# An attention and feed-forward kernel: row-sum reciprocals widened by VectorE into a buffer and turned by four whole transposes

## The chip, the cores and the metric

The kernel runs on one core of one Trainium2 chip. The metric is the device time of one execution in microseconds. Three runs of the kernel before gave 667.19, 667.30 and 667.51 us, median 667.3 us.

## The reference, cut to what matters

```python
q_rot, k_rot = rotate(q), rotate(k)            # (4, 8, 576, 64) float32
scores = scale * q_rot @ k_rot.T               # per batch and head: 576 x 576
attn = exp(scores - max(scores))
attn = attn / (sum(attn) + 1e-9)               # one row sum for each query
x = (attn @ v) -> (2304, 512)                  # heads side by side
h = x @ w_in                                   # (2304, 2048)
g = max(h, 0) + alpha * min(h, 0)
out = g @ w_out                                # (2304, 512)
```

## The kernel before, in words

There are two stages: attention up to about 260 us of the profile, and then the feed-forward products, chunk by chunk. The change is in attention alone.

**Pairs and periods.** Two heads are worked on together; 4 batches of 4 such pairs give 16 pairs. The code counts periods, `p` = 0 to 16. In period p the scores of pair p are computed, the probabilities of pair p are begun to be turned, and the rest of pair p-1 (its turned probabilities, its product with the values, its division by the row sums) is finished. Period 0 has no earlier pair, period 16 no pair of its own. Batches 1 and 2 (periods 4 to 11) run in a loop on all engines but TensorE.

**Tiles.** A pair has 9 score tiles of 128 rows by 576 keys: tile 0 holds the 64 last queries of both heads (`REM_TILE`), tiles 1 to 4 (`A_TILES`) the others of the first head, 5 to 8 (`B_TILES`) those of the second. TensorE computes a tile (`score`, L598) into one of two pairs of PSUM banks. VectorE copies it to SBUF and takes the row minimum of the negated scores (`maxima`, L996). ScalarE takes the exponential and the row sum into a column of `rsum` (`exps`, L828). A tile's banks are free again once its `maxima` is done.

**Units in four banks.** Everything that TensorE turns goes through four PSUM banks in a fixed order of 15 units in each period (`UNITS`, `BANK_OF`). `fill` waits until the unit that was in the bank before has been taken out (the semaphore `evac` of that bank), TensorE fills it, and ScalarE or VectorE takes it out: `flat` (L871 on ScalarE, L1046 on VectorE), `hi` (L847, ScalarE), `lo` (L1021 and L1026, VectorE). `U_MIXED` and `U_INV` follow one another in bank 2, so `U_INV` can't begin before `lo(p, U_MIXED, t)` is done.

**The row sums.** At the start of period p VectorE adds 1e-9 to the nine row sums of pair p-1 (`reciprocals` step 0, L1056) and takes the reciprocal (step 1, L1060) into `inv`, [128 queries, parity, 9 tiles]. To divide, the reciprocals are needed along the free dimension, the same in each of the 64 rows of a head. In `spread`, unit `U_INV`, TensorE gets this with 8 products: the stationary operand is one column of `inv` read 64 times (a step of zero), the moving operand is the 128x128 identity, and the output is one head's half of the bank (L647). The two halves `HEADS` are the two column groups of the array. ScalarE copies the bank to `inv_sb`, and `normalise` (L1071, VectorE) multiplies the product with the values (`pv`, L696 and L700) by it. Tile 0's reciprocals go through `U_MIXED` (L655) and L1026.

**Order.** Each engine runs its own list in order; nothing is reordered between engines but by semaphores. TensorE's period is: KQREM, score 0, QREM, KREM, PB0-1, scores 1 and 2, PB2-3, Q, K, scores 3 and 4, MIXED, `pv` half 0, scores 5 and 6, INV, PA0-1, scores 7 and 8, PA2-3, `pv` half 1. `pv` half 1 reuses the bank of half 0 and waits until `normalise` of half 0 is done.

**GpSimd** rotates the queries and keys of later pairs (`rope`: L453 twice, L458, L462, all with SBUF operands), and in periods 4 to 11 splits `w_in` beside it (L468, L475). L458 on the queries waits until TensorE has done `U_MIXED` (L655).

Of the kernel before, what the change touches and what calls it, by code (L numbers as in the profile page):

```python
# [8 lines left out]
ALU = mybir.AluOpType  # L9
# [3 lines left out]
P = 128  # L13
# [20 lines left out]
def build(nc, q, k, v, w_in, w_out, alpha, cos, sin, eye, out):  # L34
# [27 lines left out]
    def has_prev(p):  # L62
        return not (isinstance(p, int) and p <= 0)
# [34 lines left out]
    def unit_count(p, u):  # L98
        return tally(p, u, range(UNITS))
# [43 lines left out]
    with ExitStack() as ctx:  # L143
        used = [0]

        def sb(stack, name, shape, dt=F32):
            used[0] += -(-4 * int(np.prod(shape[1:])) // 32) * 32
            return stack.enter_context(nc.sbuf_tensor(name, shape, dt))

        def sem(name):  # L150
            return ctx.enter_context(nc.semaphore(name))
# [17 lines left out]
        with ExitStack() as att:  # L169
            rot_q = sb(att, "rot_q", [P, ST, P])  # L170
            rot_k = sb(att, "rot_k", [P, ST, P])
            cos_sb = sb(att, "cos_sb", [P, ST, D])
            sin_sb = sb(att, "sin_sb", [P, ST, D])
            q_nat, q_swap, k_nat, k_swap = [], [], [], []
            for i in range(2):
                q_nat.append(sb(att, f"q_nat{i}", [P, 2, QT * P + P], F32R))
                if i == 0:
                    early = used[0]
            for i in range(2):
                q_swap.append(sb(att, f"q_swap{i}", [P, 2, QT * P], F32R))  # L180
                k_nat.append(sb(att, f"k_nat{i}", [P, 2, REM + S], F32R))
                k_swap.append(sb(att, f"k_swap{i}", [P, 2, HALF], F32R))
            under_w_out = 4 * (2 * CT * CHUNK + FT * DM + 2 * CHUNK)
            sb(att, "behind_scores", [P, (under_w_out - used[0]) // 4])
            of_scores = used[0]
            raw_v = [sb(att, f"raw_v{i}", [P, ST, P]) for i in range(2)]
            sb(att, "behind_values", [P, CT * CHUNK - 2 * ST * P])


            until_prob = used[0]  # L190
            prob = sb(att, "prob", [P, QT, 2 * S])
            prob_rem = sb(att, "prob_rem", [P, S])

            pt = sb(att, "pt", [P, 3 * QT + 1, S])
            inv_sb = sb(att, "inv_sb", [P, S])
            nmax = sb(att, "nmax", [P, 2, TILES])
            rsum = sb(att, "rsum", [P, 2, TILES])
            inv = sb(att, "inv", [P, 2, TILES])
            ident = sb(att, "ident", [P, P])
            zero = sb(att, "zero", [P, 1])  # L200
            tiny = sb(att, "tiny", [P, 1])
            blank = sb(att, "blank", [P, P])
# [67 lines left out]
        evac = [sem(f"evac{i}") for i in range(T_BANKS)]  # L270
        sum_done = sem("sum_done")
        inv_done = sem("inv_done")
        pv_done = sem("pv_done")
        x_done = sem("x_done")
        w_in_high = sem("w_in_high")
# [33 lines left out]
        def is_opening(p):  # L309
            return isinstance(p, int) and p == 0  # L310
# [224 lines left out]
        def _(pe):  # L535
# [92 lines left out]
            def spread(p, t, u):  # L628

                if not exists_now(p, u):  # L630
                    return
                bank = fill(p, u)
                if u == U_KQREM:
                    pe.wait_ge(exp_done, (p - 1) * TILES + 1)
                elif u != U_INV and has_next(p):
                    turned_in(p, 1)
                if u != U_KQREM and has_prev(p):
                    pe.wait_ge(inv_done, p)
                pe.sem_inc(pair_filled, 1)
                par = (t - 1) % 2  # L640
                if u == U_KQREM:
                    for r in HEADS:
                        mm = nc.tensor.matmul(bank[r, 0:REM], prob_rem[:, QT * P:S], ident[:, r], start=True, stop=True)  # L643
                elif u == U_INV:
                    for i in range(QT):
                        for r, n in zip(HEADS, (A_TILES[i], B_TILES[i])):
                            mm = nc.tensor.matmul(bank[r, i * P:(i + 1) * P], inv[:, par, n:n + 1].to_broadcast([P, D]),  # L647
                                                  ident[:, :], start=True, stop=True)
                else:
                    if has_next(p):  # L650
                        for r in HEADS:
                            mm = nc.tensor.matmul(bank[r, 0:P], rot_q[:, QT, r], ident[:, :], start=True, stop=True)  # L652
                    if has_prev(p):
                        for r in HEADS:
                            mm = nc.tensor.matmul(bank[r, P:P + REM], inv[:, par, 0:1].to_broadcast([P, D]),  # L655
                                                  ident[:, r], start=True, stop=True)
                mm.then_inc(turned, 1)
# [324 lines left out]
        def _(dve):  # L982

            def maxima(p, t, n):

                if not has_now(p):
                    return
                dve.wait_ge(scored, p * TILES + (n + 1))
                if has_prev(p):
                    if n == REM_TILE:  # L990
                        dve.wait_ge(turned, unit_count(p, U_QREM))
                    elif n == A_TILES[0]:
                        dve.wait_ge(turned, unit_count(p, U_KREM))
                    elif n == B_TILES[0]:
                        dve.wait_ge(turned, unit_count(p, U_PB[-1]))
                nc.vector.tensor_scalar(row_of(n), s_ps[(t * TILES + n) % 2], -SCALE, None, ALU.mult, ALU.min,  # L996
                                        accum_out=nmax[:, t % 2, n:n + 1]).then_inc(max_done, 1)
# [48 lines left out]
                    ins = nc.vector.tensor_copy(dst, src)  # L1046
                ins.then_inc(evac[BANK_OF[u]], 1)

            def reciprocals(p, t, step):

                if not has_prev(p):
                    return
                par = (t - 1) % 2
                if step == 0:
                    dve.wait_ge(exp_done, p * TILES)
                    nc.vector.tensor_tensor(rsum[:, par, :], rsum[:, par, :], tiny[:, :].to_broadcast([P, TILES]),  # L1056
                                            ALU.add).then_inc(sum_done, 1)
                else:
                    dve.wait_ge(sum_done, p)
                    nc.vector.reciprocal(inv[:, par, :], rsum[:, par, :]).then_inc(inv_done, 1)  # L1060

            def normalise(p, b, t, h):

                if not has_prev(p):
                    return
                n = (p - 1) * 2 + h
                dve.wait_ge(pv_done, n + 1)
                if h == 0:
                    dve.wait_ge(evac[BANK_OF[U_INV]], evac_count(p, U_INV))
                half = slice(h * HALF, (h + 1) * HALF)  # L1070
                nc.vector.tensor_tensor(x[:, t, bass.ds(b * S + h * HALF, HALF)], value_bank(p, h), inv_sb[:, half],  # L1071
                                        ALU.mult).then_inc(x_done, 1)
# [38 lines left out]
            def period(b, t):  # L1111

                p = b * PAIRS + t
                before = (b if t else b - 1, (t - 1) % PAIRS)
                reciprocals(p, t, 0)
                flat(p, U_KQREM, t)
                maxima(p, t, REM_TILE)
                reciprocals(p, t, 1)
                flat(p, U_PB[1], t)
                maxima(p, t, A_TILES[0])  # L1120
                maxima(p, t, A_TILES[1])
                flat(p, U_PB[3], t)
                if not has_now(p):
                    dve.wait_ge(alpha_in, 16)
                    gate(0, 0, 0)
                    low_w_out(0)
                maxima(p, t, A_TILES[2])
                if not is_opening(p):
                    lo(p, U_Q, t)
                if is_closing(p):  # L1130
                    for j in range(CT):
                        split_x(0, 0, j)
                if not is_opening(p):
                    lo(p, U_K, t)
                maxima(p, t, A_TILES[3])
                if not is_opening(p):
                    lo(p, U_MIXED, t)
                maxima(p, t, B_TILES[0])
                maxima(p, t, B_TILES[1])
                if is_opening(p):  # L1140
                    for u in OF_NEW:
                        lo(p, u, t)
                normalise(p, *before, 0)
                maxima(p, t, B_TILES[2])
                maxima(p, t, B_TILES[3])
                flat(p, U_PA[2], t)
                normalise(p, *before, 1)

            nc.vector.memset(blank[:, :], 0.0).then_inc(blank_done, 1)
# [71 lines left out]
```

## Time and profile before

| | |
|---|---|
| median of the three runs | 667.3 us |
| the profiled execution | 667.3 us, its span 665.5 us |
| TensorE (PE) | 654.6 us busy, 98% |
| VectorE (DVE) | 338.2 us busy, 51% |
| ScalarE (ACT) | 320.3 us busy, 48% |
| GpSimd (POOL) | 266.8 us busy, 40% |
| granted TensorE clock, mean | 0.995 |

Between the first and last recorded instruction lie 665.5 us; 1.8 us of the execution lie around it. PE is TensorE's products and transposes, PEld its loading of the stationary operand, which overlaps. An fp32 product leaves two records of its matmul, a transpose or an fp32r product one. Ends of matmuls are modelled, so on PE the distance from start to start is read and not the duration.

### The profile page before, as it was taken

How to read it: one execution, taken by the hardware profiler on the slowest of the kernel's cores; microseconds unless marked ns; L12 is line 12 of the kernel's file. 1: busy time of each engine (PE TensorE's matmuls, PEld its weight loads, DVE VectorE, ACT ScalarE, POOL GpSimd, SP SyncE). 2: the span in 40 equal slices, each digit the busy share in tenths (PEclk: the TensorE clock that was granted, in tenths of full speed). 3: DMA queues.
4: the chain of work that ended last, by engine and by line, in shares of the span. 5: the costliest groups of instructions: out<-in, count | busy, mean ns of one | idle time of the engine just before them, and what ended most of it. 6: DMA issues, size and time to landing. Idle time of an engine off the chain costs nothing.

```text
span 665.5 us, 14995 instructions
## 1 busy us (share of the span) xinstructions
PE 654.6 (98%) x5570; PEld 561.9 (84%) x5570; DVE 338.2 (51%) x779; ACT 320.3 (48%) x730; POOL 266.8 (40%) x254
## 2 busy tenths in 40 slices
PE   7899999999999999999999999999999999999998
PEld 6787778778877777988899999999999999999996
DVE  4577887778887773456423332333233323332222
ACT  2688888888888884333332223222322232223223
POOL 3756788888776214222222222222222222222222
PEclk9799999999999999999999999999999999999999
DMA  6596455445545426000010001000100010001001
GB/s 150 147 230 175 112 127 134 116 105 121 119 107 118 97 91 253 1 0 1 1 49 0 1 0 48 1 1 0 47 0 0 0 47 0 0 0 48 1 0 48
DMA packets 73309, 41.58 MB, mean 62 GB/s; under 512 B 59812, under 2 KB 64292, under 8 KB 72740
## 3 DMA queue, kind: packets, MB, share of 16 engines
q1 hardware_dynamic: 72978, 40.62, 23.3%
q8 instruction: 40, 0.66, 0.4%
q10 hardware_dynamic: 274, 0.16, 0.1%
q14 instruction: 17, 0.14, 0.1%
HBM read 22.95 MB, written 4.72 MB: 42 GB/s over the span
## 4 chain that ended last, share of the span: by engine, by line
PE 96%; DVE 1%; ACT 1%; DMA 0%; SPq 0%; issue 0%; POOL 0%; DVEq 0%
PE banks L756 30%; PE banks L785 30%; PE banks L700 9%; PE banks L598 9%; PE banks L674 5%; PE banks L625 3%; PE banks L696 3%; PE banks L572 2%; PE banks L647 2%; PE banks L652 1%; PE banks L553 1%; DMA cos_sb<-in_cos 0%; PE banks L580 0%; PE banks L655 0%; PE banks L643 0%
## 5 line engine op out<-in xcount | busy, mean ns | idle before, releaser
L520 POOL TENSOR_TENSOR g_lo<-g,g_hi 128x384 fp32r<-128x384 f32 (+1 forms) x98 | 99.7, 1017 | 304.8 <-ACT g_hi L941 301.5
L1105 DVE TENSOR_SCALAR g<-banks,alpha_sb 128x384 f32<-128x384 f32 (+1 forms) x98 | 59.7, 609 | 249.2 <-ACT pos L932 249.2
L756 PE MATMUL banks<-x_hi,w_in_lo 128*128 128x384 f32 x384 | 129.3, 337 | 0.0
L756 PE MATMUL banks<-x_hi,w_in_hi 128*128 128x384 f32 x384 | 129.3, 337 | 0.0
L756 PE MATMUL banks<-x_lo,w_in_hi 128*128 128x384 f32 x384 | 129.0, 336 | 0.0
L932 ACT ACTIVATE pos<-banks 128x384 f32<-128x384 f32 x96 | 47.2, 491 | 169.2 <-PE banks L756 169.2
L785 PE MATMUL banks<-w_out_hi,g_hi 128*128 128x512 f32 x288 | 114.9, 399 | 0.3
L785 PE MATMUL banks<-w_out_hi,g_lo 128*128 128x512 f32 x288 | 112.9, 392 | 0.0
L785 PE MATMUL banks<-w_out_lo,g_hi 128*128 128x512 f32 x288 | 111.9, 389 | 0.0
L941 ACT ACTIVATE g_hi<-g 128x384 fp32r<-128x384 f32 (+1 forms) x98 | 50.9, 519 | 116.5 <-DVE g L1108 116.5
L828 ACT ACTIVATE prob<-prob,nmax 128x576 f32<-128x576 f32 x128 | 98.3, 773 | 1.3 <-DVE prob L996 1.1
L996 DVE TENSOR_SCALAR_CACHE_REDUCE prob<-banks 128x576 f32<-128x576 f32 x128 | 92.8, 751 | 9.6 <-PE banks L598 8.1
L756 PEld LDWEIGHTS banks<-x_hi,w_in_hi 128*128 128x128 f32 x384 | 72.2, 188 | 3.8
L756 PEld LDWEIGHTS banks<-x_lo,w_in_hi 128*128 128x128 f32 x384 | 72.2, 188 | 3.5
L871 ACT ACTIVATE pt<-banks 128x512 f32<-128x512 f32 x112 | 61.6, 595 | 25.0 <-PE banks L625 19.9
L756 PEld LDWEIGHTS banks<-x_hi,w_in_lo 128*128 128x128 f32 x384 | 72.2, 188 | 0.0
L598 PE MATMUL banks<-k_nat,q_nat 64*128 64x288 f32 x375 | 68.4, 314 | 0.1
L598 PE MATMUL banks<-k_swap,q_swap 64*128 64x288 f32 x375 | 67.7, 312 | 0.0
L700 PE MATMUL banks<-pt,raw_v 128*64 128x288 f32 x512 | 67.6, 406 | 0.0
L785 PEld LDWEIGHTS banks<-w_out_hi,g_lo 128*128 128x128 f32 x288 | 54.0, 187 | 13.8
L785 PEld LDWEIGHTS banks<-w_out_hi,g_hi 128*128 128x128 f32 x288 | 54.0, 188 | 10.0 <-issue 1.8
L785 PEld LDWEIGHTS banks<-w_out_lo,g_hi 128*128 128x128 f32 x288 | 54.1, 188 | 8.4
(80 smaller groups left out, 918.2 us busy)
## 6 DMA issues: line engine op xcount, KB each, us to landing
q_swap<-q_nat SPq DMA_DIRECT2D x32, 256.0 KB, 3.8
k_swap<-k_nat SPq DMA_DIRECT2D x32, 144.0 KB, 3.2
out<-stage SPq DMA_DIRECT2D x18, 256.0 KB, 2.0
raw_q<-in_q SPq DMA_DIRECT2D x32, 128.0 KB, 2.9
raw_k<-in_k SPq DMA_DIRECT2D x32, 128.0 KB, 2.6
raw_v<-in_v SPq DMA_DIRECT2D x32, 128.0 KB, 2.3
w_in_raw<-in_moe_w_in SPq DMA_DIRECT2D x4, 1024.0 KB, 6.9
w_out_raw<-in_moe_w_out SPq DMA_DIRECT2D x8, 512.0 KB, 6.9
```

Source lines behind the costliest of these rows:

```text
L520: nc.gpsimd.tensor_tensor(g_lo[f % 2][:, part], g[f % 2][:, part], g_hi[f % 2][:, part].bitcast(F32), ALU.subtract).then_inc(g_lo_done, 1)
L598: mm = nc.tensor.matmul(tile[:, h, :], q_of[rows, qx, of_q], k_of[rows, kx, keys], start=(j == 0), stop=(j == len(SPLIT) - 1))
L674: mm = nc.tensor.transpose(bank[:, to:to + D], prob[r, i, first + w * P:first + (w + 1) * P], ident[r, r])
L700: mm = nc.tensor.matmul(o[own, :], raw_v[par][:, j, own], pt[:, pt_slot(par, head, j), cols], start=False, stop=(j == QT - 1))
L756: mm = nc.tensor.matmul(h_ps[f % 2], w[:, j, cols], xx[:, j, :], start=(step == 0), stop=(step == 3 * CT - 1))
L785: mm = nc.tensor.matmul(y_ps[c % 2][m], lhs[j][f % 2][:, m * P:(m + 1) * P], rhs[j][:, f, :], start=(f == 0 and j == 0), stop=(f == FT - 1 ...
L828: nc.scalar.activation(row_of(n), row_of(n), ACT.Exp, scale=-1.0, bias=nmax[:, t % 2, n:n + 1], accum_out=rsum[:, t % 2, n:n + 1]).then_in ...
L871: ins = nc.scalar.activation(dst, src, ACT.Copy)
L932: nc.scalar.activation(pos[f % 2][:, :], h_ps[f % 2], ACT.Relu).then_inc(pos_done, 1)
L941: nc.scalar.activation(g_hi[f % 2][:, part], g[f % 2][:, part], ACT.Copy).then_inc(g_hi_done, 1)
L996: nc.vector.tensor_scalar(row_of(n), s_ps[(t * TILES + n) % 2], -SCALE, None, ALU.mult, ALU.min, accum_out=nmax[:, t % 2, n:n + 1]).then_i ...
L1105: nc.vector.tensor_scalar(g[f % 2][:, part], h_ps[f % 2][:, part], 0.0, alpha_sb[:, f:f + 1], ALU.min, ALU.mult).then_inc(neg_done, 1)
```

## The change

VectorE now treats the row sums in two parts. `first_sums(p, t, ...)` handles tiles 0 to 4 of pair p in period p itself; `last_sums(p, t, ...)` handles tiles 5 to 8 of pair p-1 in period p, at the places of the old `reciprocals` for its steps 0 and 1. Each has a third step, a `tensor_copy` that writes four columns of `inv`, each read 64 times, into its half (`LOW` or `HIGH`) of the new buffer `inv_wide`, [128, 4, 128]. Unit `U_INV` then is four transposes of a whole 128x128 block of `inv_wide`. `inv_wide` takes the place of a gap in SBUF behind `raw_v`.

```diff
-            def reciprocals(p, t, step):
+            def first_sums(p, t, step):
+                if not has_now(p):
+                    return
+                par, n = t % 2, p * 2 + 1
+                tiles = slice(REM_TILE, B_TILES[0])
+                if step == 0:
+                    dve.wait_ge(exp_done, p * TILES + B_TILES[0])
+                    nc.vector.tensor_tensor(rsum[:, par, tiles], rsum[:, par, tiles],
+                                            tiny[:, :].to_broadcast([P, B_TILES[0]]), ALU.add).then_inc(sum_done, 1)
+                elif step == 1:
+                    dve.wait_ge(sum_done, n)
+                    nc.vector.reciprocal(inv[:, par, tiles], rsum[:, par, tiles]).then_inc(inv_done, 1)
+                else:
+                    dve.wait_ge(inv_done, n)
+                    if has_prev(p):
+                        dve.wait_ge(turned, unit_count(p, U_INV))
+                    nc.vector.tensor_copy(inv_wide[:, :, LOW], inv[:, par, A_TILES[0]:B_TILES[0]].unsqueeze(2)
+                                          .to_broadcast([P, QT, D])).then_inc(wide_done, 1)
+            def last_sums(p, t, step):
...
+                    nc.vector.tensor_copy(inv_wide[:, :, HIGH], inv[:, par, tiles].unsqueeze(2)
+                                          .to_broadcast([P, QT, D])).then_inc(wide_done, 1)
@@ spread (TensorE)
-                if u != U_KQREM and has_prev(p):
-                    pe.wait_ge(inv_done, p)
+                if u == U_INV:
+                    pe.wait_ge(wide_done, p * 2)
+                elif u == U_MIXED and has_prev(p):
+                    pe.wait_ge(inv_done, p * 2 - 1)
...
-                        for r, n in zip(HEADS, (A_TILES[i], B_TILES[i])):
-                            mm = nc.tensor.matmul(bank[r, i * P:(i + 1) * P], inv[:, par, n:n + 1].to_broadcast([P, D]),
-                                                  ident[:, :], start=True, stop=True)
+                        mm = nc.tensor.transpose(bank[:, i * P:(i + 1) * P], inv_wide[:, i, :], ident[:, :])
@@ period (VectorE)
-                reciprocals(p, t, 0)
+                last_sums(p, t, 0)
...
-                reciprocals(p, t, 1)
+                last_sums(p, t, 1)
...
                 maxima(p, t, A_TILES[3])
+                last_sums(p, t, 2)
                 if not is_opening(p):
                     lo(p, U_MIXED, t)
                 maxima(p, t, B_TILES[0])
...
+                first_sums(p, t, 0)
+                first_sums(p, t, 1)
                 normalise(p, *before, 0)
                 maxima(p, t, B_TILES[2])
                 maxima(p, t, B_TILES[3])
                 flat(p, U_PA[2], t)
+                first_sums(p, t, 2)
                 normalise(p, *before, 1)
```

## Rows read from the trace of the kernel before

**Rows 1.** The page: granted clock by slice, chain that ended last by engine
```profile
PEclk9799999999999999999999999999999999999999
...
PE 96%; DVE 1%; ACT 1%; DMA 0%; SPq 0%; issue 0%; POOL 0%; DVEq 0%
```

**Rows 2.** The chain within 119 to 134 us: start us, us on it, what
```profile
128.13 1.02 PE banks L647 x16
```

**Rows 3.** Timeline of PE in periods 7 and 8: start us, us, instruction
```profile
128.06 1.09 PE L647 MATMUL banks<-ident,inv 128*64 128x128 f32 x16
129.09 0.71 PE L674 MATMUL banks<-ident,prob 64*128 64x64 f32 x16
129.61 0.37 PE L598 MATMUL banks<-k_swap,q_swap 64*128 64x288 f32 x1
...
131.18 0.71 PE L696 MATMUL banks<-pt,raw_v 128*64 128x288 f32 x4
...
142.78 1.09 PE L647 MATMUL banks<-ident,inv 128*64 128x128 f32 x16
```

**Rows 4.** Timeline of DVE in period 7, with idle before and its releaser
```profile
126.58 0.45 DVE L1021 TENSOR_TENSOR q_nat<-banks,q_nat 64x64 fp32r<-64x64 f32 x2
...
127.26 0.21 DVE L1026 COPY inv_sb<-banks 128x64 f32<-128x64 f32 x1
127.77 0.76 DVE L996 TENSOR_SCALAR_CACHE_REDUCE prob<-banks 128x576 f32<-128x576 f32 x1 [0.30 <-PE banks L598]
...
129.13 0.08 DVE L996 DVE_READ_ACCUMULATOR prob<-banks 128x1 f32 x1
130.03 0.46 DVE L1071 TENSOR_TENSOR x<-banks,inv_sb 128x288 f32 x1 [0.81 <-ACT inv_sb L871]
...
133.99 0.46 DVE L1071 TENSOR_TENSOR x<-banks,inv_sb 128x288 f32 x1 [1.55 <-PE banks L700]
```

**Rows 5.** Timeline of POOL in periods 6 and 7
```profile
118.98 1.47 POOL L468 TENSOR_TENSOR w_in_hi<-w_in_raw,zero 128x768 f32 x1
...
124.80 1.56 POOL L458 TENSOR_TENSOR rot_q<-raw_q,cos_sb 128x640 f32<-128x640 f32 x1 [2.41 <-PE banks L655]
126.44 1.56 POOL L462 TENSOR_TENSOR rot_q<-rot_q,swapped 128x640 f32<-128x640 f32 x1
127.96 1.81 POOL L475 TENSOR_TENSOR w_in_lo<-w_in_raw,w_in_hi  x1
129.73 1.44 POOL L453 TENSOR_TENSOR swapped<-raw_k,sin_sb 128x256 f32<-128x256 f32 x2
```

**Rows 6.** Row-sum instructions: L1056 and L1060, all 16 (min/median/max ns); then one
```profile
L1056 DVE TENSOR_TENSOR rsum<-rsum,tiny x16: 169/636/746, 31.7 to 252.2; 128x9 f32<-128x9 f32 x16
...
L1060 DVE RECIPROCAL inv<-rsum x16: 197/208/211, 33.0 to 252.9; 128x9 f32<-128x9 f32 x16
...
119.73 0.75 DVE L1056 TENSOR_TENSOR rsum<-rsum,tiny 128x9 f32<-128x9 f32 x1
```

**Rows 7.** Timeline at 75 us: POOL twice without a pause, DVE beside it
```profile
75.42 1.70 POOL L453 TENSOR_TENSOR swapped<-raw_q,sin_sb 128x320 f32<-128x320 f32 x2 [0.83 <-DMA raw_q<-in_k]
75.58 0.74 DVE L1056 TENSOR_TENSOR rsum<-rsum,tiny 128x9 f32<-128x9 f32 x1
```

**Rows 8.** SBUF-only VectorE instructions of 384 elements: min/median/max ns
```profile
L1087 DVE CAST x_hi<-x x20: 350/354/354, 296.4 to 588.7; 128x384 fp32r x16, 128x384 fp32r<-128x384 f32 x4
...
L1089 DVE TENSOR_TENSOR x_lo<-x,x_hi x20: 557/558/559, 296.8 to 589.1; 128x384 fp32r<-128x384 f32 x20
```

**Rows 9.** POOL's L462 and DVE's L1021 in periods 2 and 13
```profile
52.78 1.55 POOL L462 TENSOR_TENSOR rot_q<-rot_q,swapped 128x640 f32<-128x640 f32 x1
...
52.91 0.45 DVE L1021 TENSOR_TENSOR q_nat<-banks,q_nat 64x64 fp32r<-64x64 f32 x2
...
214.82 1.55 POOL L462 TENSOR_TENSOR rot_q<-rot_q,swapped 128x640 f32<-128x640 f32 x1
...
214.96 0.45 DVE L1021 TENSOR_TENSOR q_nat<-banks,q_nat 64x64 fp32r<-64x64 f32 x2
```

More of the change, by code:

```diff
@@ L186, in build @@
             raw_v = [sb(att, f"raw_v{i}", [P, ST, P]) for i in range(2)]
-            sb(att, "behind_values", [P, CT * CHUNK - 2 * ST * P])
+            inv_wide = sb(att, "inv_wide", [P, QT, P])
+            assert 2 * ST + QT >= CT * MT
             until_prob = used[0]
@@ L272, in build @@
         inv_done = sem("inv_done")
+        wide_done = sem("wide_done")
         pv_done = sem("pv_done")
@@ L1051, in reciprocals @@
+            def last_sums(p, t, step):
                 if not has_prev(p):
                     return
-                par = (t - 1) % 2
+                par, n = (t - 1) % 2, p * 2
+                tiles = slice(B_TILES[0], TILES)
                 if step == 0:
                     dve.wait_ge(exp_done, p * TILES)
-                    nc.vector.tensor_tensor(rsum[:, par, :], rsum[:, par, :], tiny[:, :].to_broadcast([P, TILES]),
-                                            ALU.add).then_inc(sum_done, 1)
-                else:
-                    dve.wait_ge(sum_done, p)
-                    nc.vector.reciprocal(inv[:, par, :], rsum[:, par, :]).then_inc(inv_done, 1)
+                    nc.vector.tensor_tensor(rsum[:, par, tiles], rsum[:, par, tiles],
+                                            tiny[:, :].to_broadcast([P, QT]), ALU.add).then_inc(sum_done, 1)
+                elif step == 1:
+                    dve.wait_ge(sum_done, n)
+                    nc.vector.reciprocal(inv[:, par, tiles], rsum[:, par, tiles]).then_inc(inv_done, 1)
+                else:
+                    dve.wait_ge(inv_done, n)
+                    nc.vector.tensor_copy(inv_wide[:, :, HIGH], inv[:, par, tiles].unsqueeze(2)
+                                          .to_broadcast([P, QT, D])).then_inc(wide_done, 1)
```

## The prediction

> **What bounds the kernel now.** I read the page first. The chain that ended last is 96% TensorE, and the granted clock is at its upper level, 2.4 GHz, in all slices but the second [rows 1]; so a microsecond off TensorE's list in attention comes off the end, as long as nothing else becomes late. Then the chain in the steady part: unit INV, the 8 products of L647, is a link of it with 1.02 us [rows 2]. Period 7 stands for the others (14.72 us from INV at 128.06 to the next at 142.78). Its PE timeline has no pause about INV: the next unit, PA0-1, starts 1.03 us after it [rows 3]. Last I read what DVE and POOL do at those microseconds, since the change gives DVE three more instructions in each period and makes INV wait for one of them. Two things are to be seen there. First, DVE's list just before INV is tight: `lo` of MIXED (L1021, L1026) runs from 126.58 to 127.47, and INV, which takes the same bank, starts 0.59 us behind its end [rows 3, 4]. Second, POOL is in the middle of an instruction at that moment: L462 from 126.44 to 128.00 [rows 5].
>
> **INV on TensorE.** Removed are 8 products, 16 records in 1.03 us, 64 ns each. Four transposes of 128x128 come in. No row has this shape. Between the ends: PA0-1 has 16 transposes with half-height stationary blocks of 128 columns, 0.52 us from start to start, so 65 ns for two [rows 3]. If a whole transpose costs what two half-height ones cost, four take 0.26 us. To that comes a change of unit: 16 records of 128 columns at 2.4 GHz are 0.85 of INV's 1.03 us, which leaves 0.18 for it, while PA0-1 shows next to none; I allow 0.12, which makes 0.38 and a gain of 0.65. If they take as long as the 8 products, it is nothing. PA0-1's blocks have a moving side of 64 columns, the new ones 128; if the time goes by those, the unit takes 4 x 0.13 = 0.52 us. I take 0.52, a gain of 0.51 us, since that is the nearest row counted by columns. INV exists in periods 1 to 16: 16 x 0.51 = 8.2 us, between 0 and 10.4.
>
> The Trainium skill ("TensorE: Matmul & The Clock Gate", section "LDWEIGHTS (loading the stationary operand)") puts a load at its number of columns over 1.2 GHz. An estimate from this page is 107 ns for each 128-column block, 0.43 us for four, and 0.55 with the change of unit: it agrees with the value taken to 0.03 us.
>
> **The two adds and two reciprocals.** The add (L1056) takes 169 ns at least, the reciprocal 197 to 211 [rows 6]. For `last_sums` they only get shorter, at their old places. For `first_sums` they are new, 0.17 + 0.2 us, and stand where DVE waits 0.81 us for ScalarE to take INV out, ahead of `normalise` half 0 [rows 4].
> The add has a second price, though. Its median is 636 ns with 9 elements, and the row at 119.73 says why: it ends at 120.48, and POOL's L468 ran from 118.98 to 120.45 [rows 5, 6]. At 75.58 the same: it ends at 76.32, as the first of POOL's two L453 (0.85 us each, from 75.42) is over and before the second is [rows 7]. So a VectorE add with both inputs in SBUF waits for POOL's running instruction, and gets its turn ahead of POOL's next one. The new add comes when maxima 6 is done (129.21, plus the delay below), within POOL's L475 or L453: up to 0.7 us. I come to that below.
>
> **The two wide copies.** 128x256 from `inv` to `inv_wide`, both in SBUF. The nearest in size and kind is the cast L1087, 354 ns for 384 elements, where the two-input L1089 takes 558 for as many [rows 8]. Were the fixed part alike, the difference of 204 ns would be half of the 384 elements at some 1.06 ns each: the one-input form moves two at a time. So a copy of 256 is 354 - 64 x 1.06 = 0.29 us free of any wait; at one element at a time it would be 558 - 128 x 1.06, 0.42.
> Does it wait for POOL as the add does? No row shows a copy between SBUF tensors while POOL works. The nearest rows point both ways: the add waits (up to 746 ns for 9 elements), the reciprocal, SBUF to SBUF too but with one input, never does (at most 211) [rows 6]. Bounds: 0 and the rest of POOL's instruction. What decides for me is L1087's double pace: it needs a second stream out of SBUF as the add's second input does, and the reciprocal doesn't show one. I take it that the copy waits.
>
> The Trainium skill ("SBUF — State Buffer", section "Who interferes with whom") says that an fp32 copy in a 2-port mode and a GpSimd instruction hold the shared ports for their whole length, and whoever comes second stands still. The rows on the add agree for two inputs (636 against 169 ns); for the copy no run here shows it yet.
>
> **Where HIGH's copy lands.** `last_sums` step 2 stands between maxima 4 and `lo` of MIXED, so it starts where L1021 starts now, 126.58, 0.14 us after POOL's L462 began [rows 4, 5]. This is no chance of period 7: L462 is tied to TensorE's MIXED through L458, which waits for L655 [rows 5], and DVE's list is tied to the same point; in each of periods 2 to 13, 12 of them, L462 starts 0.13 to 0.18 us before L1021; the first and the last of them are shown [rows 9]. In period 1 POOL is elsewhere (its second L453, soon over), and in 14 to 16 `rope` has no L462 there.
> So in 12 periods the copy waits until 128.00, streams 128 steps (0.13 us) and ends about 128.16; the next instruction follows 0.08 earlier by the usual overlap of records, at 128.08 in place of 126.58. `lo` of MIXED ends 1.50 us later, at 128.97. TensorE has been at INV since 128.06, and starts it at about 129.03: a stall of 0.97 us. Its bounds are 0 (no wait for POOL) and 1.3 (POOL's end and the copy a little later each). 12 x 0.97 = 11.6 us. Where there's no such wait the copy's 0.21 us of start-to-start goes into the 0.30 us of DVE's pause before maxima 5 [rows 4]: nothing.
>
> **What else is late then.** Behind the copy on DVE stand `lo` of MIXED, maxima 5 and 6. Maxima 5 starts 1.13 us later and ends at 129.6; TensorE asks for it at score 7 (new 129.97); maxima 6 ends at 130.34 and score 8 asks at 130.4: just met. The add of `first_sums` comes at about 130.3. In periods 4 to 11 POOL, itself pushed back 0.15 us, is in its first L453 until 130.7; add, reciprocal and `normalise` half 0 end at 131.35, and `pv` half 1 asks at 131.54 (131.18 + 0.97 - 0.51 is 131.64, and 0.1 is kept in hand [rows 3]): met. In periods 2, 3, 12 and 13 POOL has no L475, is one instruction ahead, and the add waits for its L458 of 1.28 us: `pv` half 1 is late by some 0.13 us, 4 x 0.13 = 0.5 us. LOW's copy stands ahead of `normalise` half 1, where DVE now has 1.55 us of pause [rows 4]; waiting for POOL's L462 on the keys takes about 1.0 of it. Nothing. In periods 4 to 11 the delayed POOL then holds the next period's first add some 0.1 us longer than TensorE is late: 8 x 0.1 = 0.8 us.
>
> **Sum.** +11.6 + 0.5 + 0.8 - 8.2 = +4.7 us. The profiled execution took 667.3 us (span 665.5 and 1.8 around it), the median of the three runs too, so: 672.0 us, span 670.2. With the unit at 0.38 and the stall at 0.9 it is +1.7, with the unit at 0.7 and the stall at 1.3 about +12: 668 to 679 for this case by itself.
>
> **Rivals.**
> *The copy doesn't wait* (the other side). Place: DVE after maxima 4. The gain of INV stays whole, TensorE finds the bank free at 128.06 still. 667.3 - 8.2 = 659.1, between 657 and 662. For it: the reciprocal's row, and the margin of 0.14 us, which a POOL that begins a little later would turn round. Against: the pace of L1087, and that the margin is there in all 12 periods. It decides as soon as the stall is under 0.68 us a period (8.2/12).
> *The copy waits longer than one instruction.* If it needs more than the add does and loses its turn to the POOL instruction queued behind (L475 of 1.81 us in 8 periods, an L453 of 0.7 in 4), the stall grows by 17 us in all: 689. The row at 75 us speaks against it, for an add.
> *The transposes gain nothing* (the change doesn't do what it says), as whole blocks use the array no better than two column groups side by side. With the stall: 667.3 + 12.9 = 680.2. Against: a transpose leaves one record where a product leaves two, and PA0-1 does 16 in half the time of L647's 16 [rows 3].
>
> **Chances.** The forecast 0.68, the copy that doesn't wait 0.22, transposes without gain 0.05, the longer wait 0.05. The range from 658 to 679 us takes in the first two but for their tails. No change is what stays within 0.2% (1.3 us, about what a measurement of this kernel can tell): the forecast with the quickest transposes and the shortest stall, 0.06. Slower 0.71, faster 0.23.
>
> **What would show it.** In the profile after: a `tensor_copy` at the place after maxima 4 with a median near 1.6 us in 12 of 16 and 0.29 in the others, its end at the end of POOL's L462; PE idle ahead of the transposes, released by DVE's L1026 of `lo`, about 1 us each; transposes with 0.5 us to the next unit; periods near 15.2 us. The prediction is wrong if the copies all take 0.3 us, or if POOL's L462 now starts after them. One more thing would upset it: pauses of 1 us in each 15 that bring the granted clock down; in the second slice, where period 0 has its pauses, it is at 0.7 [rows 1].

## The result, and the profile after

| | before | after |
|---|---|---|
| median of four runs | 667.38 us (667.19 to 667.51) | 672.38 us (671.06 to 673.21) |
| ratio, 95% interval | | 1.0071 (1.0055 to 1.0088) |
| span of the profiled execution | 665.5 us | 671.4 us |

The change is slower by 5.0 us. The forecast was 672.0.

In the page, TensorE was 96% of the chain that ended last [rows 1]; now it shares it.
```profile
span 671.4 us, 14700 instructions
PE 649.2 (97%) x5378; PEld 554.7 (83%) x5378; DVE 368.9 (55%) x843; ACT 320.5 (48%) x730; POOL 267.8 (40%) x254
...
PE 80%; DVE 13%; issue 5%; ACT 1%; DMA 0%; SPq 0%; DVEq 0%; POOL 0%
```
TensorE does less (649.2 us busy), and the span is longer all the same. The timeline of one period shows where it went, first POOL and DVE about HIGH's copy (L1086), then PE. These answer to [rows 3], [rows 4] and [rows 5].
```profile
128.10 1.56 POOL L460 TENSOR_TENSOR rot_q<-raw_q,cos_sb 128x640 f32<-128x640 f32 x1 [2.80 <-PE banks L657]
129.74 1.55 POOL L464 TENSOR_TENSOR rot_q<-rot_q,swapped 128x640 f32<-128x640 f32 x1
131.25 1.86 POOL L477 TENSOR_TENSOR w_in_lo<-w_in_raw,w_in_hi  x1
...
129.95 1.49 DVE L1086 COPY inv_wide<-inv 128x256 f32<-128x256 f32 x1
131.36 0.45 DVE L1023 TENSOR_TENSOR q_nat<-banks,q_nat 64x64 fp32r<-64x64 f32 x2
...
132.03 0.21 DVE L1028 COPY inv_sb<-banks 128x64 f32<-128x64 f32 x1
...
132.39 0.63 PE L650 MATMUL banks<-ident,inv_wide 128*128 128x128 f32 x4 [0.95 <-DVE inv_sb L1028]
132.95 0.71 PE L676 MATMUL banks<-ident,prob 64*128 64x64 f32 x16
...
147.64 0.63 PE L650 MATMUL banks<-ident,inv_wide 128*128 128x128 f32 x4 [0.96 <-DVE inv_sb L1028]
```
The copy starts 0.21 us after POOL's L464 and ends 0.15 us after it; `lo` of MIXED (L1023, L1028) comes behind it; TensorE stands idle for 0.95 us until L1028 is done, then runs the four transposes with 0.56 us to the next unit, where the products took 1.03. From INV to INV it is 15.25 us, before 14.72.

The copies' own line (min/median/max ns) shows both prices: 0.28 us free, 1.5 behind POOL.
```profile
L1068 DVE COPY inv_wide<-inv x16: 281/765/1400, 30.6 to 256.9; 128x256 f32<-128x256 f32 x16
L1086 DVE COPY inv_wide<-inv x16: 284/1496/1566, 38.5 to 266.7; 128x256 f32<-128x256 f32 x16
```
LOW's copies (L1068) are long in part too, but stand in the pause ahead of `normalise` half 1; no TensorE wait is put down to them. The same view of the transposes (L650):
```profile
L650 PE MATMUL banks<-ident,inv_wide x64: 272/273/329, 40.8 to 268.5; 128*128 128x128 f32 x64
its engine sat idle before it (us, times) until:
  issue: 15.8, 16
  DVE inv_sb L1028: 12.4, 13
```
The line `issue` belongs to the loading of the stationary operand (PEld) and isn't a pause of PE. The last line is TensorE's: its pauses ahead of INV that DVE's L1028 ended, 12.4 us in 13 periods. Against them stand 16 units shorter by 0.47, 7.5 us. 12.4 - 7.5 = 4.9, and the medians differ by 5.0. The spans of the two profiled executions differ by 5.9, 1.0 more than that sum; 0.4 of it lies in periods 2 to 13 (see the small terms below).

### The profile page after: what moved, and what is told of

Same layout as the page of the kernel before. It is cut to its first block, busy times and chain, and to the rows that moved or that the text cites. A ratio compares the mean times of both kernels' runs of the same rounds, so it can differ in the third digit from the quotient of the medians.

```text
span 671.4 us, 14700 instructions
## 1 busy us (share of the span) xinstructions
PE 649.2 (97%) x5378; PEld 554.7 (83%) x5378; DVE 368.9 (55%) x843; ACT 320.5 (48%) x730; POOL 267.8 (40%) x254
## 4 chain that ended last, share of the span: by engine, by line
PE 80%; DVE 13%; issue 5%; ACT 1%; DMA 0%; SPq 0%; DVEq 0%; POOL 0%
PE banks L758 30%; PE banks L787 30%; PE banks L702 5%; PE banks L676 3%; DVE prob L998 3%; PE banks L600 3%; DVE inv_wide L1086 3%; PE banks L574 2%; DVE pt L1048 2%; PE banks L698 2%; DVE k_nat L1023 2%; PE banks L650 1%; PE banks L627 1%; DVE q_nat L1023 1%; DVE prob_rem L998 1%
```

## The experiments

Each median is compared with runs of the kernel before on the same chip; these were at 667.5 to 667.6. Executions of one kernel here lie up to 4.4 us apart, wider than in the first runs. The granted clock goes with it: of the kernel before, the five executions with a mean clock of 1.00 took 665.6 to 665.9 us, the three with 0.989 or 0.990 took 669.4 to 670.0. The low stretches lie at the start: between 20 and 40 us the clock is 0.71 and then 0.95 in the changed kernel's profiled execution, and in that of the first experiment it is 0.83 between 10 and 20 us and 1.00 from there. The later periods run at 1.00, so their lengths are free of it.

**HIGH's copy moved.**
```diff
                 flat(p, U_PB[3], t)
+                last_sums(p, t, 2)
...
                 maxima(p, t, A_TILES[3])
-                last_sums(p, t, 2)
```


> The changed kernel with one line moved: HIGH's copy stands behind flat of PB3 instead of behind maxima 4, where GpSimd pauses for TensorE's MIXED in most periods. Theory (the copy waits for GpSimd's running instruction, and TensorE's INV waits behind it): the 13 long copies become 0.3 us, TensorE's pause of 0.96 us ahead of INV goes, 672.4 - 13 x 0.95 = about 660 us. Rival (it is the work added to VectorE that is late, wherever it stands): 672, as the list is as long as before.

Measured: 664.32 us, ratio 0.9955 (0.9938 to 0.9972). The same instructions in another order are 8 us faster than the changed kernel, so it isn't the amount of work on VectorE. HIGH's copies are free now:
```profile
L1086 DVE COPY inv_wide<-inv x16: 280/283/403, 34.8 to 255.4; 128x256 f32<-128x256 f32 x16
```
The same view of the transposes (L650) has no line left for a pause that DVE ended. But 4 us of what I expected are missing. Outside GpSimd's split of `w_in` periods are 14.3 us (53.68 to 67.98), within it 14.76 (126.57 to 141.33). The timeline there:
```profile
132.27 1.46 POOL L470 TENSOR_TENSOR w_in_hi<-w_in_raw,zero 128x768 f32 x1
...
132.62 1.14 DVE L1079 TENSOR_TENSOR rsum<-rsum,tiny 128x4 f32<-128x4 f32 x1
133.68 0.21 DVE L1048 COPY pt<-banks 128x64 f32<-128x64 f32 x1
...
133.24 0.41 PE L627 MATMUL banks<-ident,prob 64*128 64x64 f32 x8
133.99 0.68 PE L676 MATMUL banks<-ident,prob 64*128 64x64 f32 x15 [0.33 <-issue]
```
The add of four elements now comes just after POOL has begun L470 and takes 1.14 us. PB0-1 (L676), which needs the bank that L1048 empties, is late. The period after the first INV is as long (38.87 to 53.68), so there are 8 long ones, 3.7 of the 4 us. In the kernel before the same add waited too (median 0.64 us, 0.75 at most [rows 6]); here it is 0.89 and up to 1.25. That VectorE then had to wait for TensorE anyway is shown by the run that changes this add alone, further down.

**Wide reciprocals in place of the copies.**
```diff
-                    dve.wait_ge(inv_done, n)
-                    nc.vector.tensor_copy(inv_wide[:, :, HIGH], inv[:, par, tiles].unsqueeze(2)
-                                          .to_broadcast([P, QT, D])).then_inc(wide_done, 1)
+                    dve.wait_ge(sum_done, n)
+                    nc.vector.reciprocal(inv_wide[:, :, HIGH], rsum[:, par, tiles].unsqueeze(2)
+                                         .to_broadcast([P, QT, D])).then_inc(wide_done, 1)
```
(and LOW's likewise, from tiles 1 to 4, its waits untouched)

> The changed kernel with both wide copies replaced, in place, by a reciprocal of the row sums read 64 times each, which writes the wide buffer directly. Theory (a one-input form that moves two elements at a time needs what GpSimd holds, a reciprocal doesn't): each takes about 0.42 us, longer than a free copy's 0.28, but never waits; TensorE's pause goes, about 660 us. Rival (anything from SBUF to SBUF waits for GpSimd): 672 to 674. Rival (the added time on VectorE is what costs): 674.

Measured: 681.47 us, ratio 1.022 (1.0199 to 1.0241). My price was wrong by four times, so the time says nothing on the rivals. The line does:
```profile
L1086 DVE RECIPROCAL inv_wide<-rsum x16: 1746/1748/1749, 37.1 to 274.4; 128x256 f32<-128x256 f32 x16
...
131.44 1.55 POOL L464 TENSOR_TENSOR rot_q<-rot_q,swapped 128x640 f32<-128x640 f32 x1
131.64 1.75 DVE L1086 RECIPROCAL inv_wide<-rsum 128x256 f32<-128x256 f32 x1
132.95 1.80 POOL L477 TENSOR_TENSOR w_in_lo<-w_in_raw,w_in_hi  x1
```
A reciprocal of 256 elements takes 1.75 us, across the end of one POOL instruction and into the next or with POOL at rest: 3 ns between the shortest and the longest. It doesn't wait; it is slow.

**GpSimd waits for the copy.**
```diff
                 pool.wait_ge(rope_step, step + 3)
+                if side == 0 and has_prev(p - 2) and not (isinstance(p, int) and p < 3):
+                    pool.wait_ge(wide_done, (p - 2) * 2)
```


> The changed kernel with one wait added on GpSimd: its last add on the queries (the one that HIGH's copy runs into) starts after HIGH's copy. VectorE's list is untouched. Theory: the copy finds GpSimd idle and takes 0.3 us, GpSimd is 0.2 to 0.5 us later and has room for it; about 661 us (660 to 663). Rival (VectorE's added work costs by itself): 672.

Measured: 666.11 us, ratio 0.9977 (0.9961 to 0.9993). VectorE's list is untouched. The copy's median is 0.29 us; one case of 0.94 is left, in period 1, where the copy meets GpSimd's instruction before that one. Period 7:
```profile
127.04 0.29 DVE L1088 COPY inv_wide<-inv 128x256 f32<-128x256 f32 x1
127.41 1.56 POOL L466 TENSOR_TENSOR rot_q<-rot_q,swapped 128x640 f32<-128x640 f32 x1 [0.65 <-DVE inv_wide L1088]
128.45 0.66 PE L652 MATMUL banks<-ident,inv_wide 128*128 128x128 f32 x4
```
It is GpSimd's instruction that held the copy. The run is worth 6 us and not the 11 expected: GpSimd is 0.65 us later, and the add of `first_sums`, which stands ahead of `normalise` half 0, now has a median of 1.08 us (0.31 in the changed kernel). The view of waits has TensorE's `pv` half 1 waiting for `normalise` in 8 periods, 2.8 us in all. That is part of the missing 5 us; the rest is not followed.

**The eight products with the copies kept.**
```diff
-                        mm = nc.tensor.transpose(bank[:, i * P:(i + 1) * P], inv_wide[:, i, :], ident[:, :])
+                        for r, n in zip(HEADS, (A_TILES[i], B_TILES[i])):
+                            mm = nc.tensor.matmul(bank[r, i * P:(i + 1) * P], inv[:, par, n:n + 1].to_broadcast([P, D]),
+                                                  ident[:, :], start=True, stop=True)
```


> The changed kernel, both copies and all their waits kept, but INV done by the eight old products from inv instead of the four transposes. It prices the transposes alone. Theory (a unit of 0.56 us in place of 1.03): 672.4 + 16 x 0.47 = about 680 us. Rival (TensorE waits there anyway and the unit's length is hidden by the pause or given back later): 672 to 674.

Measured: 679.52 us, ratio 1.0175 (1.0158 to 1.0192), 7.1 us over the changed kernel. 16 x 0.47 are 7.5; here the pause stands in 12 periods and not 13, which takes off 0.8. The pause comes ahead of the unit, so the unit's length counts in full, within the executions' spread:
```profile
135.30 1.09 PE L651 MATMUL banks<-ident,inv 128*64 128x128 f32 x16 [0.96 <-DVE inv_sb L1030]
136.32 0.71 PE L678 MATMUL banks<-ident,prob 64*128 64x64 f32 x16
```

**Copies one element at a time.** The place is as in the changed kernel, the form is that of `maxima`.
```diff
-                    nc.vector.tensor_copy(inv_wide[:, :, HIGH], inv[:, par, tiles].unsqueeze(2)
-                                          .to_broadcast([P, QT, D])).then_inc(wide_done, 1)
+                    nc.vector.tensor_scalar(inv_wide[:, :, HIGH], inv[:, par, tiles].unsqueeze(2)
+                                            .to_broadcast([P, QT, D]), 1.0, None, ALU.mult, ALU.min,
+                                            accum_out=scrap[:, 0:1]).then_inc(wide_done, 1)
```
(LOW's likewise)

> The changed kernel with both wide copies, in place, written as a tensor_scalar (times 1.0) that also keeps a minimum in its accumulator, the form of maxima. It has one input and should move one element at a time. Theory (only a form that moves two at a time, or has two SBUF inputs, waits for GpSimd): about 0.42 us each and never more, TensorE's pause ahead of INV goes. The first add of the next period is left to run into GpSimd as in the run with the copy moved, so the time is that run's, about 664.5 us (663 to 666). Rival (any copy out of SBUF waits): 672.

Measured: 664.37 us, ratio 0.9949 (0.9933 to 0.9965).
```profile
L1088 DVE TENSOR_SCALAR_CACHE_REDUCE inv_wide<-inv x16: 412/416/419, 39.2 to 257.9; 128x256 f32<-128x256 f32 x16
...
126.08 1.56 POOL L465 TENSOR_TENSOR rot_q<-rot_q,swapped 128x640 f32<-128x640 f32 x1
126.22 0.42 DVE L1088 TENSOR_SCALAR_CACHE_REDUCE inv_wide<-inv 128x256 f32<-128x256 f32 x1
...
127.70 0.66 PE L651 MATMUL banks<-ident,inv_wide 128*128 128x128 f32 x4
```
Same 256 elements, same place, POOL's instruction begun 0.14 us before as ever, and it takes 0.42 us in all 16 cases. An instruction slower by 0.13 us than a copy that is free made the kernel 8 us faster. This is the run that tells that the form decides, not the place or the operands. The form differs from the copy in two things, the pace and the accumulator. The reciprocal, which has no accumulator, doesn't wait either, so an accumulator isn't needed for that; that the pace is the cause is the simplest reading of both, and no run changes it alone.

**The copy moved, and the adds in that form too.**
```diff
-                    nc.vector.tensor_tensor(rsum[:, par, tiles], rsum[:, par, tiles],
-                                            tiny[:, :].to_broadcast([P, QT]), ALU.add).then_inc(sum_done, 1)
+                    nc.vector.tensor_scalar(rsum[:, par, tiles], rsum[:, par, tiles], 1e-9, None, ALU.add, ALU.min,
+                                            accum_out=scrap[:, 3:4]).then_inc(sum_done, 1)
```
(the add of `first_sums` likewise; HIGH's copy as in the first run)

> The kernel with HIGH's copy moved, and the two adds of 1e-9 in the one-input form with accumulator in place of the add with two SBUF inputs. Theory (in the run with the copy moved, the add at the start of a period waits up to 1.14 us for GpSimd and holds up TensorE by about 0.46 us in each of periods 4 to 11): 664.3 - 8 x 0.46 = about 660.6 us, all periods 14.3 us. Rival (the longer periods come from something else in GpSimd's split of w_in): 664.

Measured: 661.87 us, ratio 0.9919 (0.9893 to 0.9945). POOL runs L471 as before, from 131.84 to 133.31, and the add beside it takes 0.16:
```profile
131.84 1.47 POOL L471 TENSOR_TENSOR w_in_hi<-w_in_raw,zero 128x768 f32 x1
132.27 0.16 DVE L1080 TENSOR_SCALAR_CACHE_REDUCE rsum<-rsum 128x4 f32<-128x4 f32 x1
```
Periods 4 to 11 are 14.28 us each on the mean (83.27 to 197.54 in 8), the same as outside. In the run with the copy moved that stretch took 117.65 us (82.26 to 199.91), here 114.27, so the 0.46 us were the add's. The medians give 2.5 us of the 3.7 expected.

**Copies and adds in that form, VectorE's order untouched.** The edits of the two runs before, HIGH's copy at its place.

> The changed kernel with VectorE's order untouched, both copies and both adds in the one-input form with accumulator: nothing of the row sums can wait for GpSimd. Theory: about 660.6 us; the whole of the transposes' gain of about 7.5 us less almost nothing. Rival (the longer copies, 0.42 us against 0.28, on VectorE's tight list cost something): 661 to 663.

Measured: 661.71 us, ratio 0.9901 (0.9863 to 0.9939). From period 2 to period 13 it is 14.28 us a period (56.05 to 213.17 in 11). This and the run before are the fastest versions; their intervals overlap. The time lies in the range of the rival, but the run before, whose copies of HIGH have a median of 0.28 us, has the same periods and the same time. So nothing shows a cost of the longer copies. In this trace TensorE also stands still for 0.86 us at 50.3 us, which no other trace has; no view gives its cause.

**The kernel before with its add in that form.** The same edit, nine elements.

> The kernel before with only its add of 1e-9 in the one-input form with accumulator. Its add waits for GpSimd too (median 636 ns), but VectorE then waits for TensorE anyway. Theory: no change, 667.0 to 667.8 us, the add at about 0.2 us. Rival (that wait cost something all along): 8 x 0.4 less, about 664.

Measured: 667.44 us, ratio 0.9995 (0.9979 to 1.0011). The add is 164 ns in place of 636 and nothing comes of it:
```profile
L1057 DVE TENSOR_SCALAR_CACHE_REDUCE rsum<-rsum x16: 163/164/167, 33.5 to 254.4; 128x9 f32<-128x9 f32 x16
```
The view of waits says where the time went: between 80 and 200 us VectorE's maxima 0 now waits for TensorE in 8 periods, 4.5 us in all, and in the kernel before once, 0.3 us. So the wait was hidden in the kernel before. It came out when TensorE's list was shorter and the add met more of GpSimd's instruction; the runs don't part these two.

**No contention, and the eight products.** Both copies and both adds in that form, with the products of the fourth run.

> The kernel in which nothing of the row sums can wait for GpSimd (both copies and both adds in the one-input form with accumulator), with INV done by the eight old products instead of the four transposes. It prices two things: against the same kernel with transposes (661.7) the transposes where nothing hides them, against the kernel before (667.5) all of VectorE's added work when it never waits. Theory: the added 1.3 us a period on VectorE lie in its pauses and cost nothing, so periods are 14.72 us as before and the time is 667.5 to 668.5; the transposes are worth 16 x 0.47 = 7.5 us or a little less. Rival (the added work costs in part by itself): periods over 14.8 us, 669 or more.

Measured: 667.19 us, ratio 1.0 (0.9984 to 1.0015). From 53.46 to 215.29, 11 periods, 14.71 us each, as before. So all that the change adds to VectorE costs nothing once it doesn't wait, and against 661.71 the transposes are worth 5.5 us by the medians. By the period it is 0.43 to 0.47 us, 16 of which are 6.9 to 7.5. The difference lies within the executions' spread: the one execution of each at a mean clock of 1.00 took 664.95 and 658.87 us, 6.1 apart, and the profiled execution of the run with the transposes has the pause of 0.86 us in it.

## Why the prediction was right

- **INV on TensorE.** 0.56 us to the next unit, 0.52 predicted: 0.47 saved in place of 0.51, 7.5 us in place of 8.2. In the period of 132 us the four start at 132.39, 132.53, 132.64 and 132.75, so 0.11 us apart but for the first, and the next unit comes 0.20 us after the last. The value taken, 4 x 0.13, had no change of unit in it: a block was priced too high and the change of unit at nothing, and the two nearly cancel, which is luck. The working beside it, 107 ns for a block and 0.12 for the change of unit, has the parts nearer. A block of the loading itself is recorded with 0.14 us, so the loads overlap.
- **The copy's own price** was 0.28 us, 0.29 predicted. That it waits for POOL, the step for which rows pointed both ways, was right: 1.49 against a worked-out 1.58. The pace of the cast [rows 8] was the right row to decide by. The wide reciprocal and the one-at-a-time copy, 16 instructions each without a wait, show it from the other side. The Trainium skill ("SBUF — State Buffer", section "Who interferes with whom") has both sides of it: a copy or a `tensor_scalar` can enter a 2-port mode and then contends with GpSimd, and the `tensor_scalar` that also writes out its accumulator doesn't enter one. These runs agree: 1.5 us against 0.28 for the copy, 0.41 to 0.42 in all 32 cases of the other form.
- **The stall.** 0.96 us a period, 0.97 predicted. It struck 13 periods and not 12: I had left out period 1 because POOL was in its second L453 there. In the profiled execution that pair came 0.3 us earlier (36.49 against 36.82), POOL had begun the next instruction at 38.13, and the copy came at 38.45 and took 1.40. What GpSimd does there hangs on a transfer, not on TensorE, and could not be counted on; in the run with the eight products and the copies kept, period 1 has no pause. This term was 0.8 us too small (12.4 against 11.6), the gain of the transposes 0.7 too large, and the small terms below too large. That the forecast came within 0.4 us of the median is in part these errors against one another.
- **The small terms** (+0.5 and +0.8) were too large. In the period of 132 us the first half's add took 0.30 us, and TensorE showed no wait of its own there; 15.25 - 14.72 - 0.96 + 0.47 leaves 0.04 a period. In periods 2, 3, 12 and 13, where the prediction had the add hold up `pv` half 1, it took 0.53 to 0.59 us and TensorE waited for nothing of it. From the first INV to the thirteenth it is 183.17 us, before 176.80; the stalls less the shorter units are 5.9 of these 6.4, so 0.4 us are left where the prediction had 1.3, at most 0.10 in any period. I have not followed where they lie.
- **Which of the rivals fell.** The copy that doesn't wait: by the trace after. Transposes without gain: by the two runs with the products. The wait longer than one instruction: the copy ends 0.15 us after L464 though L477 stands ready, as the add's row had it [rows 7].
- **What the sum hadn't.** The contention of the add was in the prediction as a wait and priced at 0.1 us a period, which was fair for the changed kernel, whose TensorE stands still anyway. It was 0.46 in 8 periods as soon as the copy's stall was out of the way, so a repair of the copy alone brings 3 us below the kernel before and not 6.

## What to carry to other kernels

A VectorE instruction that adds two SBUF tensors, or copies from SBUF to SBUF two elements at a time, can take as long as what is left of the GpSimd instruction that it meets; before adding one, look at what GpSimd does at the microsecond where it will start, and at what is queued behind it. The slower form may be the faster kernel: one input with an accumulator, 0.42 us for 256 elements and never more in these runs. After such a repair look at all other instructions of the same kind, since waits that were hidden come out one by one as the bound engine's list gets shorter.

## What the runs showed that I had not expected

- VectorE's reciprocal from SBUF takes 170 ns for 4 elements, 190 for 5, 208 for 9 and 1748 for 256, some 6.2 ns for each beyond the ninth. Up to 9 elements that looks like any other small instruction, and I had priced the wide one at 0.42 us.
- A `tensor_scalar` with an accumulator on four elements takes 0.16 us beside a GpSimd instruction in which the two-input add took 1.14.
